# Three sets of load buffers, outputs three groups behind and a subtraction on GpSimd in an unrolled linear-attention stage

## The reference

```python
def _attn_ref(q, k, v, phi):                      # all 8 x 8 x 576 x 64, phi 8 x 8 x 576 x 32
    a = phi - np.max(phi, axis=2, keepdims=True)  # softmax over the 576 positions
    a = np.exp(a)
    a = a / (np.sum(a, axis=2, keepdims=True) + 1e-09)
    k_m = np.einsum('bhsm,bhsd->bhmd', a, k)      # 32 memory rows of k and of v
    v_m = np.einsum('bhsm,bhsd->bhmd', a, v)
    scores = scale * np.matmul(q, k_m.transpose(0, 1, 3, 2))
    scores = scores - np.max(scores, axis=-1, keepdims=True)
    attn = np.exp(scores)
    attn = attn / (np.sum(attn, axis=-1, keepdims=True) + 1e-09)
    return np.matmul(attn, v_m)

def _moe_ref(x, w_in, w_out):                     # x is 4608 x 512, d_ff 2048
    h = x @ w_in
    g = h * (1.0 / (1.0 + np.exp(-1.702 * h)))
    return g @ w_out

def reference(...):
    x = attention, heads side by side: 4608 x 512
    x = _moe_ref(x, ...)
    return _moe2_ref(x, ...)                      # 8 experts, each token goes to one
```

## Time and profile before

| | us |
|---|---|
| median of three runs | 1368.81 |
| lowest and highest | 1366.98 and 1371.24 |
| the profiled execution | 1368.63 |
| its span, first to last instruction | 1367.0 |
| attention (to the first matmul of the dense stage) | about 117 |

### The profile page before, as it was taken

The page is one execution under the profiler, slowest core; times in us unless marked ns, Lnnn a source line. Parts: engine busy times, 40 slices in busy tenths (PEclk is TensorE's granted clock), DMA queues, the critical chain, the costliest instruction groups (busy, mean ns, idle before and its releaser), DMA issues.

```text
span 1367.0 us, 23811 instructions
## 1 busy us (share of the span) xinstructions
PE 1317.9 (96%) x6866; PEld 1056.9 (77%) x6867; DVE 635.1 (46%) x1291; ACT 390.8 (29%) x725; POOL 549.2 (40%) x648
## 2 busy tenths in 40 slices
PE   5888899999999999999999999999999999999997
PEld 3445688888888888888888888887788888888886
DVE  4776243353343433534334344346655555555553
ACT  3564122222222222322222222223332222232221
POOL 2335683353454433443444334511533343433332
PEclk9899999999999999999999999999999999999999
DMA  8897437556566465465654646547884789648882
GB/s 316 319 352 304 156 130 210 192 184 183 189 213 179 169 192 190 151 189 177 180 187 163 192 172 173 177 159 261 228 229 101 202 228 268 177 118 254 251 245 63
DMA packets 152376, 274.19 MB, mean 201 GB/s; under 512 B 16916, under 2 KB 54053, under 8 KB 149765
## 3 DMA queue, kind: packets, MB, share of 16 engines
q1 hardware_dynamic: 94468, 196.04, 43.2%
q10 hardware_dynamic: 44672, 45.63, 13.2%
q0 software_dynamic: 13184, 31.88, 7.5%
HBM read 144.98 MB, written 100.45 MB: 180 GB/s over the span
## 4 chain that ended last, share of the span: by engine, by line
PE 85%; DMA 3%; POOL 1%; issue 1%; DVE 1%; ACT 0%; ACTq 0%; POOLq 0%
PE ps L702 28%; PE ps L734 28%; PE ps L804 14%; PE ps L775 14%; DMA raw<-in_moe_w_in 2%; PE ps L744 1%; DMA cq<-ch 1%; DMA cmeta<-record_scratch 0%; POOL W L1550 0%; ACTq L1036 0%; DVE chT L1371 0%; POOL W L1548 0%; DVE cqT L1358 0%; POOL out L1663 0%; POOL W L1540 0%
## 5 line engine op out<-in xcount | busy, mean ns | idle before, releaser
L702 PE MATMUL ps<-xs,W 128*128 (+1 forms) x1728 | 419.2, 391 | 3.0 <-POOL W L1550 3.0
L734 PE MATMUL ps<-W,gs 128*128 128x512 f32 x1728 | 417.0, 390 | 4.3 <-POOL W L1540 4.2
L734 PEld LDWEIGHTS ps<-W,gs 128*128 128x128 f32 x1728 | 325.2, 188 | 73.1 <-issue 5.0
L702 PEld LDWEIGHTS ps<-xs,W 128*128 128x128 f32 x1728 | 324.0, 188 | 73.3 <-issue 6.5
L1234 DVE TENSOR_TENSOR gate<-ps,gate 128x512 f32<-128x512 f32 x144 | 99.6, 692 | 373.0 <-ACT gate L978 370.4
L978 ACT ACTIVATE gate<-ps 128x512 f32<-128x512 f32 x144 | 86.2, 598 | 477.6 <-PE ps L702 453.4
L804 PE MATMUL ps<-W,chT 128*128 (+1 forms) x936 | 218.4, 389 | 2.5 <-DVE chT L1371 2.5
L775 PE MATMUL ps<-W,cx 128*128 (+1 forms) x936 | 218.6, 389 | 0.8 <-issue 0.8
L1604 POOL CAST whi<-raw 128x512 fp32r<-128x512 f32 x128 | 82.9, 648 | 331.4 <-DMA raw<-in_moe_w 331.4
L804 PEld LDWEIGHTS ps<-W,chT 128*128 128x128 f32 x936 | 175.5, 188 | 39.9 <-issue 3.6
L775 PEld LDWEIGHTS ps<-W,cx 128*128 128x128 f32 x936 | 175.5, 188 | 37.8 <-issue 1.4
(11 more groups left out here) (163 smaller groups left out, 786.1 us busy)
## 6 DMA issues: line engine op xcount, KB each, us to landing
W<-expert_scratch SPq DMA_DIRECT2D x24, 2048.0 KB, 11.2
raw<-in_moe_w SPq DMA_DIRECT2D x128, 256.0 KB, 2.8
expert_scratch<-whi SPq DMA_DIRECT2D x128, 256.0 KB, 2.6
expert_scratch<-raw SPq DMA_DIRECT2D x128, 256.0 KB, 2.9
cq<-ch ACTq DMA_DIRECT2D x156, 128.0 KB
kvm<-in_kv SPq DMA_DIRECT2D x16, 1152.0 KB, 7.3
crec<-record_scratch POOLq DMA_DIRECT2D x160, 64.0 KB
qT<-in_q SPq DMA_DIRECT2D x16, 576.0 KB, 5.1
```

The lines of the kernel that those rows point to most:

```text
L702: mm = pe.matmul(ps[:, f % 2, :], W[:, col:col + P], xs[:, bass.ds(x0 + (x_lo * K1 + c) * T, T)], start=(c == 0 and w_lo + x_lo == 0), sto ...
L734: mm = pe.matmul(ps[:, 2 + s, :], gs[:, f % 2, g_lo, s * P:(s + 1) * P], w_out_sb[:, f, w_lo, :], start=(f == 0 and g_lo + w_lo == 0), sto ...
```

## The change

- Attention is written out for all 16 groups. There are three sets of load buffers (`g % 3`), so each load waits for a group three back and not two.
- `pT` has two buffers. PE makes the output halves of group g - 3 in round g, not of g - 2. The halves of the last three groups come behind the last group, between the first matmuls of the dense stage.
- The subtraction of the scores' maximum goes from DVE to POOL (`less_max`) in all groups but the last. POOL's round is: normalize g - 2, subtract g - 1, blocks of v_m for g.
- The split of weight pieces 0 to 3 goes from groups 2, 3, 12, 13 to groups 5, 6, 9, 10, and their loads with it.
- The stores of `keep` go from ACT to SP, where they stand behind all loads of the attention and behind weight pieces 4 and 5, and ahead of piece 6: batches 0 to 4 in two transfers of 2880 KB, then batches 5 and 6 in two of 576 KB each. Batch 6 waits for the copy of group 13's output.
- Tile 0's rows of x are prepared over the last two groups (two chunks in each), not all in the last.
- The `wait` plus a register increment that the loop needs (`hold`, L417 rows) is gone where the waits are constants.

```diff
-            def load_phi(g, b, u):
-                wait(sp, s_aT, g - 1)
-                sp.dma_start(phT[u][:], phi[bass.ds(g * P, P), :]).then_inc(s_phi[u], 16)
+            def load_phi(g):
+                wait(sp, s_aT, g - 2)
+                sp.dma_start(phT[g % 3][:], phi[g * P:(g + 1) * P, :]).then_inc(s_phi[g % 3], 16)
...
+            load_kv(0)
+            load_q(0)
+            for g in range(1, NG):
+                load_phi(g)
+                load_kv(g)
+                load_q(g)
+                if g in QUARTER:
+                    c = QUARTER.index(g)
+                    load_w(c, w_in_part(c, 0))
             load_w(K1, w_out_v[0])
             load_w(K1 + 1, w_in_part(0, 1))
+            store_kept(0, FIRST, s_xfirst)
+            for b in range(FIRST, KEPT):
+                store_kept(b, 1, s_xkept)
...
-                if has_out:
-                    out_half(g - 2, (r + 2) % 4, 0)
+                if g >= 3:
+                    out_half(g - 3, 0)
...
+            out_half(NG - 3, 0)
             mm1(0, 0)
+            out_half(NG - 3, 1)
+            out_half(NG - 2, 0)
+            mm1(0, 1)
+            out_half(NG - 2, 1)
             for i in range(2):
-                out_half(NG - 2, (NG - 2) % 4, i, (4, 2)[i])
-            mm1(0, 1)
-            for i in range(2):
-                out_half(NG - 1, (NG - 1) % 4, i, (6, 4)[i])
+                out_half(NG - 1, i, (6, 4)[i])
             mm1(0, 2)
...
                 dve.tensor_reduce(scs[:, u, 0, 0:SB], by_m(u), AX.X, ALU.max).then_inc(s_dv, 1)
-                wait(dve, s_dv, DVE_A * g + 3)
-                dve.tensor_tensor(by_m(u), by_m(u), each_m(u, 0), ALU.subtract).then_inc(s_mx, 1)
...
+            def less_max(g, u):
+                pool.wait_ge(s_dv, DVE_A * (g + 1))
+                by_m = sc[u][:].rearrange("p (n m) -> p n m", m=M)
+                pool.tensor_tensor(by_m, by_m, scs[:, u, 0:1, 0:SB].rearrange("p o n -> p n o").broadcast_to([P, SB, M]),
+                                   ALU.subtract).then_inc(s_mx, 1)
...
                 if g >= 2:
                     normalize(g - 2, g % 2)
-                if g == NG - 1:
+                if g:
+                    less_max(g - 1, 1 - g % 2)
+                v_blocks(g, g % 4)
+                if g in QUARTER:
+                    c = QUARTER.index(g)
+                    split_w_in(c, c, 0)
+                if g == NG - 2:
                     for c in range(2):
                         first_x_lo(c)
```

More of the change, by code:

```diff
@@ L233, in build @@
         s_cst2 = sem("consts_loaded_by_pool")
[L234 to L236 removed]
+        s_phi = [sem(f"phi_loaded{u}") for u in range(3)]
+        s_q = [sem(f"q_loaded{u}") for u in range(3)]
+        s_kvl = [sem(f"kv_loaded{u}") for u in range(3)]
         s_amax = sem("phi_max")
@@ L632, in a_transposes, with group @@
                 tr.then_inc(s_atr, 1)
-            def group(g, b, r):
-                u = r % 2
-                has_out = not isinstance(g, int) or g >= 2
-                last = isinstance(g, int) and g == NG - 1
-                wait(pe, s_kvl[u], 16 * (b + 1))
-                if not isinstance(g, int) or g >= 3:
-                    wait(pe, s_xo, 2 * g - 5)
-                hold(pe, s_am, g + 1)
+            def group(g):
+                u = g % 3
+                pe.wait_ge(s_kvl[u], 16 * (g // 3 + 1))
+                wait(pe, s_xo, 2 * (g - 4) + 1)
+                pe.wait_ge(s_am, g + 1)
                 out_of = lambda h: ps[h * M:(h + 1) * M, 4, 3 * P:4 * P].rearrange("p (w d) -> p w d", w=2)
@@ L654, in group @@
                 mm.then_inc(s_kv, 1)
-                if not last:
+                if g + 1 < NG:
                     a_transposes(g + 1)
                 wait(pe, s_kmT, g)
-                hold(pe, s_kk, g + 1)
+                pe.wait_ge(s_kk, g + 1)
                 for i in range(2):
@@ L677, in group @@
                 mm.then_inc(s_sc, 1)
-                if has_out:
-                    out_half(g - 2, (r + 2) % 4, 1)
-            wait(pe, s_cst, 2 * 16)
+                if g >= 3:
+                    out_half(g - 3, 1)
+            pe.wait_ge(s_cst, 2 * 16)
             a_transposes(0)
-            groups(pe, group)
+            for g in range(NG):
+                group(g)
             def mm1(t, f):
@@ L1187, in x_lo, with group @@
                                   ALU.subtract).then_inc(b_xlo, 1)
-            def group(g, b, r):
-                u = r % 2
-                last = isinstance(g, int) and g == NG - 1
-                two = not isinstance(g, int) or g >= 2
-                if not last:
-                    phi_in(g + 1, b + u, 1 - u)
-                inverses(g, u, two, True)
-                if not isinstance(g, int) or g:
-                    less_max(g - 1, 1 - u)
-                if two:
-                    attn_out(g - 2, u)
+            def group(g):
+                u = g % 2
+                if g + 1 < NG:
+                    phi_in(g + 1)
+                inverses(g, u, g >= 2, True)
+                if g:
+                    scores_max(g - 1, 1 - u)
+                if g >= 2:
+                    attn_out(g - 2)
             dve.memset(padrec[:], 0.0).then_inc(b_setup, 1)
@@ L1216, in _ @@
             dve.wait_ge(s_cst, 2 * 16)
-            groups(dve, group)
+            for g in range(NG):
+                group(g)
             dve.wait_ge(b_xhi, K1)
```

198 lines of the change are left out of this document (88 added, 110 removed).

## The result

| | before | changed |
|---|---|---|
| median us (lowest to highest) | 1370.03 (1366.98 to 1373.23), 4 runs | 1348.76 (1347.78 to 1349.92), 4 runs |
| profiled execution: time / span | 1368.63 / 1367.0 | 1348.79 / 1347.1 |
| start of the row from which PE runs without a gap | 148.64 | 129.10 |

The ratio is 0.9845, with a 95% interval of 0.9819 to 0.9870: 1.5% faster. It lies in the predicted range (1344 to 1363), 5.8 us under the predicted 1354.6, and inside the rival "the deep queue runs as from 12 to 18" (1342 to 1350). The span fell by 19.9 us. The row that the prediction hung the time on came 19.5 us earlier, so what moved is where it was expected, and more than forecast.

A forecast was written before the change was run, and what follows sets the result against it. DMA was taken to set the start of PE's gapless row at 148.64 us; 5.9 us from faster loads and 8 from the closed hole and order made 14.0, so 1368.6 - 14.0 = 1354.6 us, range 1344 to 1363.

The forecast's parts named there:

- the deep queue runs as from 12 to 18: Rival on the attention's loads: 425 GB/s, loads end at 88.2 us, time 1342.7 us (1342 to 1350); chance 0.20.
- What bounds the kernel: Dense stage: time is the start of PE's gapless row at 148.64 us plus an unchanged rest; DMA sets that start.
- Loads with a third set: Attention, 20 us on: loads one group further ahead run at 362 GB/s and end at 100.1 us, not 106; 5.9 gained.
- a deeper queue can't fill engines that are full: Attention loads: the reason for taking 337 / 0.93 = 362 GB/s as the rate at full share.
- Stores on SP: Behind the loads: stores follow without a hole, piece 6 behind them lands at 120.9 us; 8 us from hole and order.
- The wait costs nothing: Last store on SP: group 13's output comes at 112 to 113 us, while batch 5's store runs until 117.
- From piece 6 to the dense stage: Weight pieces 6 to 11: four splits of 1.97, two loads of 2.68 and 0.5 for a store: 13.7 us, to 134.6.
- Compute in time: Attention's end: last scores at 105.5 us, PE needs 24.5 more and is ready at 130.0, 4.6 before the weights.
- The subtraction: Attention loop, on POOL: 1159 ns, a round of 4.86 us covered by DMA's 5.7 with 0.8 margin; nothing counted.
- The clock: PE's row at 148.64 us took 4.34, not 2.72, after its wait; new wait about as long, so that cost stays.
- The forecast's own case: Whole kernel: the time lands at 1350 to 1358 us; chance 0.45.
- three of four rows lie there: Attention loads: support for 362 GB/s, near the 358 of the stretch 20 to 32 us (share 0.98).

The follow-up runs named there:

- e4: The changed kernel with the stores of the kept outputs issued by ACT again, as before: 1351.2 us, ratio 0.9859.
- i1: The changed kernel with stores and weight pieces in turn on SP behind the group loads: 1347.1 us, ratio 0.9835.
- i2: i1 with the 1 MB load of `x2x` moved behind the pieces of the next quarter: 1343.9 us, ratio 0.9815.
- e2: The changed kernel with the maximum subtracted by DVE again in every group, not POOL: 1348.0 us, ratio 0.9838.
- u1: The changed kernel with three parts undone together (subtraction on DVE, outputs two groups behind, stores issued by ACT): 1353.2 us, ratio 0.9882.
- e3: The changed kernel with the outputs two groups behind again instead of three, in PE's and ACT's order: 1347.3 us, ratio 0.9827.
- e8_phi_two: The changed kernel with only the wait ahead of phi set back: phi two groups ahead, kv and q three: 1347.2 us, ratio 0.9839.

## Why the prediction was right, and where its sizes were off

**What bounds the kernel: right.** Time minus the start of mm1(0,4) is 1368.6 - 148.6 = 1220.0 before and 1348.8 - 129.1 = 1219.7 changed, in times of the profiled executions. In e4 it is 1351.6 - 131.9 = 1219.7. In i1, with its second wait, it is more: 1347.6 - 123.6 = 1224.0.

**Loads with a third set: mechanism right, the rate mis-sized.** The failed step is the sentence "a deeper queue can't fill engines that are full", with 337 / 0.93 = 362 taken from it. Measured: 411 from 20 to 90, and the last load (piece 5) landed at 92.1, not 100.1. That is 8.0 us, more than the whole error. In the kernel before that piece landed at 108.3, so by landings the loads came 16.2 us earlier, where 5.9 was forecast, and only 3.3 of the 19.5 us are left for everything behind them. The rival's 425 was nearer; its counter-argument (compute idle from 12 to 18) fell, since PE was busy 89% of 20 to 90 beside 411. The rival's loads would have ended at 88.2: 411 is not 425, and the changed kernel had a dip at 54 to 58 (300, 405, 273 and 245 GB/s in its four windows), whose cause no run shows. The page that the prediction set against the change (SBUF — State Buffer, Summary, in the Trainium skill, 358 GB/s) would have kept the loads at the slow end; the 423 and 424 of single stretches speak against it. Another page of the Trainium skill, Perfetto Trace Analysis, Engine Utilization, says that a core may pull more than that share when only one core of its pair is active, up to about 435: the trace agrees, and I had not weighed it.

**Stores on SP: hole closed, its worth too high.** From the loads' end to piece 6 I forecast 20.8 us (100.1 to 120.9); it took 21.4 (92.1 to 113.5), so the sum of bytes was right. But of the 14.0 I gave 8 to this part. Undone alone it costs 2.5 us: the hole it closes is now 5 us and not 8, and the same edit puts piece 6 behind the stores. I named that cost and then priced the part without an alternative in which piece 6 goes beside them. "The wait costs nothing" held: with DMA at a share of 1.01 from 100 to 110, SP's wait for the last copy emptied nothing.

**From piece 6 to the dense stage: 13.7 forecast, 15.6 measured.** The chain changed over to the odd pieces: the cast in the split of piece 7 took 1.08 (0.61 elsewhere), and the loads of 9 and 11 took 2.95 and 4.04 and not 2.68, the last beside `x2x`. I had counted all loads as on idle engines. Together: -8.0 + 0.6 + 1.9 = -5.5, and 134.6 - 5.5 = 129.1.

**Compute in time: right.** The last scores came 10.8 us behind the last phi (11.7 forecast), at 97.43. PE then needed 26.6 us (24.5 forecast) and was there before the weights, with 5.06 of idle time (4.6 forecast).

**The subtraction: right to count nothing, but its cover was thinner.** It took 1157 ns a piece with DVE at work beside it. The margin of 0.8 us a round rested on 362 GB/s; at 411 a group's 2.06 MB take 5.0 us against a loop of 4.74, and in the last five rounds the loop was the chain. With it undone the time is the same, since the slack ahead of the weights hides it. The factor of 2 in the Trainium skill (GPSIMD Engine Reference, Engine selection) is 1.47 here, 1157 / 789.

**The clock: a cost kept that grew.** I left the low-clock cost of the row behind the wait at 4.34, saying that the new wait would be about as long; the old one was 2.99. It was 5.46, after 5.06 us of idle, against 2.88 at full clock. From 129 to 134 the granted clock was 0.50, the lower level of 1.2 GHz:

```profile
129.00:134.00 5.00, 4.90 (x12) 3.87 (x13) 0.00 (x0) 0.00 (x0) 3.34 (x4) 0.50 0.37 124
```

In i2, where the wait is 0.83, the same row takes 3.01 and the clock stays at 1.00. The wait of 5 us thus costs 7.6 here. The cost does not grow with the wait: behind 5.41 us (e2) the row took 4.49 and behind 5.71 (e4) 4.60, behind 4.43 (u1) and 4.68 (e3) 5.42 and 5.46. What decides between the two, no run separates.

**Chances.** The range held. The forecast's own case (1350 to 1358) missed by 1.2 us, and the case with a chance of 0.20 came true: with two of the five rows at a share of 0.93 or more above 400 (425 and 409), "three of four rows lie there" was a weak reason to put it so low. That the forecast landed within 6 us is in part luck: its two parts, 5.9 and 8, came out as 16.2 and 3.3, and their errors went opposite ways.

## What to carry to other kernels

Read a DMA rate at full share in windows of about 1 us, not as a mean divided by its share: here the peaks between the dips were what a deeper queue then gave nearly throughout. Give the further buffer to every tile that would otherwise be released last on the queue that issues the loads (here q and kv, not phi), and count the bytes on their way at that issue. When a transfer is moved on a queue, price what then stands behind it, and the next consumer too: each gain here showed up only up to the next late transfer.

## What the runs showed of the hardware

- One core held 420 GB/s of loads from HBM for 70 us (e3_out2, e8_phi_two), each 1-us window of e3_out2 at 380 or more, with PE 89 to 90% busy. With 1.2 to 1.5 MB on their way at the issue of the load released last it was 334 to 351, with 3.3 MB 411 to 420.
- A high DMA share does not show a full rate: in the kernel before, the 1-us windows at 180 to 249 GB/s have shares of 0.55 to 0.97, and in one of them a packet of 9 KB takes 0.54 us where it takes 0.35 at 415 GB/s.
- A wait of 5.06 us on PE was followed by 5.46 us for 12 matmuls that take 2.88 at full clock, waits of 5.41 and 5.71 us by 4.49 and 4.60; a wait of 0.83, by 3.01.
